# A longer unused strip ahead of the last stage's buffers

## The reference

```python
# 1: attention, 4 x 8 heads, 768 positions, head size 64
keep = is_sink | in_window            # 4 sink keys, a window of 128
a = softmax(where(keep, q @ k.T / 8, -1e9));  x = (a @ v)   # as rows [3072, 512]
# 2: routed experts, 8 of them, F = 1024, top 1, for rows with x @ w_skip > 0
y = gate_w * (relu(x @ w1[e]) @ w2[e]);       x = x + y
# 3: dense, d_ff = 2048
h = x @ w_in;  r = maximum(h, 0);  g = r * r
out = g @ w_out                       # [3072, 512] float32
```

## The kernel before

| tile | bytes | address before | address after |
|---|---|---|---|
| `to_line` | 96, then 1504 | 218,880 | 217,472 |
| `x_hi` | 8192 | 210,688 | 209,280 |
| `x_lo` | 8192 | 202,496 | 201,088 |
| `relu_c` | 4096 | 198,400 | 196,992 |
| `g` | 4096 | 194,304 | 192,896 |
| `g_hi` | 4096 | 190,208 | 188,800 |
| `g_lo` | 4096 | 186,112 | 184,704 |

## Time and profile before

### The profile page before, as it was taken

How to read it: one execution, slowest core, us unless ns; L and a number is a source line. 1 busy time by engine, 2 the same in 40 slices (tenths; PEclk the granted TensorE clock), 3 DMA queues, 4 the chain that set the end, 5 groups by cost and what they waited for, 6 DMA issues and landing times.

```text
span 937.1 us, 16992 instructions
## 1 busy us (share of the span) xinstructions
PE 914.0 (98%) x5152; PEld 731.1 (78%) x5153; DVE 472.6 (50%) x1419; ACT 420.8 (45%) x970; POOL 81.7 (9%) x147
## 2 busy tenths in 40 slices
PE   7999999989999998999999999999999999999998
PEld 5778777767888876788888887888888888878886
DVE  5787899876666767653242234222422332242224
ACT  7888999844666667542131223111311222232122
POOL 3111111123111111100000000000000000000000
PEclk9999999989999999999999999999999999999999
DMA  5556774375666688620021003000400040004001
GB/s 197 168 164 218 222 239 152 98 282 187 233 243 225 234 309 301 234 46 1 0 63 28 1 1 85 4 0 0 90 0 0 0 90 0 0 0 90 0 0 45
DMA packets 87364, 99.52 MB, mean 106 GB/s; under 512 B 56093, under 2 KB 56221, under 8 KB 87312
## 3 DMA queue, kind: packets, MB, share of 16 engines
q1 hardware_dynamic: 81168, 83.34, 28.3%
q0 software_dynamic: 6000, 15.49, 4.9%
q10 hardware_dynamic: 144, 0.07, 0.0%
HBM read 77.72 MB, written 25.56 MB: 110 GB/s over the span
## 4 chain that ended last, share of the span: by engine, by line
PE 91%; issue 2%; ACT 2%; DVE 2%; DMA 1%; ACTq 1%; DVEq 0%; SPq 0%
PE bank L1128 29%; PE bank L1114 29%; PE bank L1029 7%; PE bank L1010 7%; PE bank L869 5%; PE bank L924 4%; PE bank L897 4%; PE bank L935 1%; PE bank L1018 1%; PE bank L949 1%; PE bank L917 1%; DMA w_raw<-in_weights 1%; PE bank L1002 1%; ACT prob L667 0%; DVE x_row L1304 0%
## 5 line engine op out<-in xcount | busy, mean ns | idle before, releaser
L1498 DVE TENSOR_TENSOR g<-relu_c 128x512 f32<-128x512 f32 x96 | 66.4, 692 | 353.9 <-ACT relu_c L812 353.8
L812 ACT ACTIVATE relu_c<-bank 128x512 f32<-128x512 f32 x96 | 57.3, 597 | 385.1 <-PE bank L1114 385.1
L1114 PE MATMUL bank<-x_hi,w_lo 128*128 128x512 f32 x384 | 151.5, 395 | 0.7 <-DVE x_lo L1485 0.7
L1128 PE MATMUL bank<-w_hi,g_lo 128*128 128x512 f32 x384 | 152.0, 396 | 0.0
L1128 PE MATMUL bank<-w_lo,g_hi 128*128 128x512 f32 x384 | 151.7, 395 | 0.0
L1114 PE MATMUL bank<-x_lo,w_hi 128*128 128x512 f32 x384 | 151.6, 395 | 0.0
L1128 PE MATMUL bank<-w_hi,g_hi 128*128 128x512 f32 x384 | 151.5, 395 | 0.0
L1114 PE MATMUL bank<-x_hi,w_hi 128*128 128x512 f32 x384 | 151.5, 395 | 0.0
L667 ACT ACTIVATE prob<-score,neg_max 128x264 f32<-128x264 f32 (+1 forms) x192 | 94.0, 496 | 15.0 <-DVE neg_max L1190 15.0
L1457 DVE TENSOR_TENSOR w_lo<-w_raw,w_hi x70 | 81.9, 1220 | 21.3 <-ACT w_hi L775 10.3
L1128 PEld LDWEIGHTS bank<-w_hi,g_lo 128*128 128x128 f32 x384 | 72.1, 188 | 18.8 <-DVE g_lo L1505 1.6
(11 more groups left out here) (149 smaller groups left out, 1282.1 us busy)
## 6 DMA issues: line engine op xcount, KB each, us to landing
w_raw<-in_weights SPq DMA_DIRECT2D x80, 512.0 KB, 5.0
k_in<-in_kT SPq DMA_DIRECT2D x24, 264.0 KB
q_in<-in_qT SPq DMA_DIRECT2D x24, 256.0 KB, 3.4
v_in<-in_v SPq DMA_DIRECT2D x24, 256.0 KB
x_rows<-x_row SPq DMA_DIRECT2D x24, 256.0 KB
x_row<-x_rows SPq DMA_DIRECT2D x96, 64.0 KB, 2.4
out<-w_raw SPq DMA_DIRECT2D x12, 512.0 KB, 2.9
x_res<-routed POOLq DMA_DIRECT2D x15, 260.0 KB, 3.3
```

Of the source, the lines that this page charges most:

```text
L1114: ins = eng.matmul(hc_ps[f % 2][:, :], w[f // UNIT][:, f % UNIT, wcols], x[:, c, :], start=(c == 0 and n == 0), stop=(c == DC - 1 and n == 2))
L1128: ins = eng.matmul(yc_ps[s][:, :], gg[:, f % 2, s * P:(s + 1) * P], w[f // UNIT][:, f % UNIT, DM:CH], start=(f == 0 and n == 0), stop=(f = ...
L1498: eng.tensor_tensor(g[:, f % 2, :], relu_c[:, f % 2, :], relu_c[:, f % 2, :], ALU.mult).then_inc(s_cg, 1)
```

## The change

The strip's length is written down as 1504 bytes; before, it was worked out as 128 - 32 = 96 bytes. The six tiles of the last stage move down by 1408 bytes. No instruction is added, removed or reordered.

```diff
-LINE = 128
+TO_LINE = 1504
...
         part_hi, part_lo, sits = hb_hi[:, 0, :], hb_lo[:, 0, :], hb_lo[:, 1, :]
-        sb("to_line", [P, (LINE - 8 * 4) // 4], F32, side="right")
+        sb("to_line", [P, TO_LINE // 4], F32, side="right")
         x_hi = sb("x_hi", [P, DC, SUPER], F32R, side="right")
```

## The result

The changed kernel takes 924.66 us (median of 4 runs, 922.68 to 927.08) against 937.44 for the kernel before on the same chip: a ratio of 0.9865, 95% interval 0.9847 to 0.9884, or 12.8 us less. The forecast was 922.2, in a range of 920.5 to 938.0. The profiled executions are 938.59 and 924.29 us, 14.3 apart.

The account below looks back on a forecast made before the run. It took TensorE's matmul spacing to bound the last stage: 15.4 us from 233.3 to 226.7 ns, less 0.6 for `g_lo` waits and 0.35 unsettled, gives 14.5 off 936.7, so 922.2 us, range 920.5 to 938.0.

Parts of the forecast that it names:

- the full gain: Last stage: both matmul lines settle at 226.7 ns; 14.5 us gained, 922.2 us (920.5 to 924.5), chance 0.50.
- the signs it named: Last stage: 2.72 us per 12 matmuls, some 441 per 100 us, durations 0.39, ScalarE's L1114 wait down about 14 us.
- TensorE's spacing bounds the last stage: Last stage: only the spacing of TensorE's matmuls sets the time, 233.3 ns each against 226.7 in the expert stage.
- The spacing comes from where the two operands lie: Last stage: operands start 128 bytes apart modulo 512; 256 apart, as in the expert stage, should save 6.6 ns each.
- The exchanged roles in `inner`: In `inner` (L1114) `x` moves and weights stand, unlike the expert stage; after the change its streams are also 256 bytes apart.
- Nothing: Rival: something other than the address keeps the last stage's spacing at 233.3 ns; time stays 936.7 us, chance 0.27.
- half: Rival: in the last stage only `outer` settles, gaining 3.2 to 7.6 us; 931.3 us, chance 0.13.
- slower: Rival: `inner`'s new address pair meets worse, 236 ns a matmul, 3.1 us lost; about 940 us, chance 0.10.
- The sum: Last stage: 15.4 us from faster spacing, less 0.6 for waits and 0.35 for unsettled matmuls, gives 14.5 us gained.
- the wait for `g_lo` at the end of a round: Last stage, `outer` at each round's end: one spacing 0.33 us in place of 0.23, 6 times, 0.6 us stays.
- The 0.2 us either way for ScalarE and VectorE: Their reads and writes of the six moved tiles: taken as 0, bounded by 0.2 us to either side.

Follow-up runs that it names:

- the run with `g_lo` first: Changed kernel with VectorE's last `lower_part` of a round moved ahead of `turn_c` for the fourth chunk: 921.38 us against the changed kernel's 923.52.
- the second timing: The changed kernel, unaltered, timed once more against the kernel before on one chip: 923.52 us against 936.73, ratio 0.9861.

## Why the prediction was right

The range of 920.5 to 938.0 us held both the full gain and no change at all, so that the time fell into it says little. What bears the prediction out is the signs it named, above all 2.72 us for 12 matmuls in both lines and 441 of them in 100 us. Its ground was one difference between two stages and its chance for the full gain 0.50; that the address was the right one among the differences was shown only by the experiments.

*TensorE's spacing bounds the last stage.* Right: groups of 12 matmuls went from 2.80 us to 2.72 and the stage shrank by 13.34 us, with nothing else changed.

*The spacing comes from where the two operands lie.* Right, and shown by moving the weights alone. The prediction was wider than it had to be: it said that only a dependence on the remainder modulo 512 or a smaller power fits, and it is the smaller power 256. What it argued from, that the rhythm doesn't follow c or s, couldn't tell the two apart, since a slice is 512 bytes. The exchanged roles in `inner`, on which it doubted, make no difference at a multiple of 256 bytes, but at 64 bytes the direction counts. The strip of 1504 bytes works because it brings the tiles to a multiple of 256 from the weights; 224 bytes do the same, and the tiles need not lie as the expert stage's do.

*Nothing, half, slower.* "Nothing" fell: the same matmuls take 2.80 or 2.72 us for 12 by placement alone. The Trainium skill (TensorE: Matmul & The Clock Gate, "Step-by-step: what each phase is for") says that loading the next tile's weights takes no read bandwidth from the running matmul. The measurement decides against the conclusion that placement therefore costs nothing; whether read bandwidth is what is lost, or something else on the way of the two operands, no run shows. "Half" exists, but only where the tiles of the two layers lie at different distances. The price named for "slower", 236 ns a matmul, was never met over a group: 2.80 us for 12 in the last stage, and 4.21 for 18 in the expert stage, are the dearest steady groups on the chain at any distance tried.

*The sum.* It gave 14.5 us for the stage; 13.34 came. The mis-sized term is the wait for `g_lo` at the end of a round, set at 0.10 us, 6 times. With faster matmuls TensorE reaches that point sooner after the round's last `inner`, while VectorE, which that `inner` sets going and which makes `g_lo` after two pieces of `x_lo` and two transposes, takes as long as before. Between the two lie the 24 matmuls of two `outer` groups; by an estimate from the spacings they take 24 x 6.6 ns = 0.16 us less, and the wait for `g_lo` grew from 1.6 to 2.5 us over 6 rounds, by 0.15 each. So the two spacings of 0.38 and 0.34 are 0.15 and 0.11 above 0.227, 6 x 0.27 = 1.6 us, where 0.6 was left. That is 1.0 of the 1.1 us missing, and the run with `g_lo` first got back 1.79 us of the stage (524.37 - 522.58). The prediction asked what the faster engine would reach too early in the middle of the round, where there are 3.5 us to spare; at its end it took the wait as it stood. The 0.2 us either way for ScalarE and VectorE held: `x_lo` still takes 674 ns.

*The time.* 922.2 stands 2.5 us below the measured 924.66, which is just outside the bounds given for the full gain (920.5 to 924.5); the second timing, 923.52, is inside. Of the 2.5, 0.7 is that the kernel before was taken at 936.7 where four runs gave 937.44, and 1.1 is the sum's. The rest is that the medians differ by 12.8 us (13.2 in the second timing, 936.73 - 923.52) where the stages differ by 13.3, which is within what the runs vary.

## What to carry to other kernels

When two stretches of the same matmul form run at the same granted clock with different spacing, and no wait on the chain explains it, compare where their stationary and moving operands start: here 6.6 ns of 233.3 hung on it, 13.3 us in 2304 matmuls, and unused bytes bought it back. For this form of matmul, place the two operands' tiles a whole number of 256 bytes apart, by a strip on one side, with slices that are multiples of that; tiles placed for one stage can spoil another that shares the weights. After a bound engine gets faster, look again at the end of each loop, where the slack is least: here what was queued ahead of the last value that it waits for was worth some 2 us.

## What the runs showed of the hardware

The spacing of 128x128 by 128x512 FP32R matmuls, each with its own weight load, settles at 226.7 ns at full clock if both operands start 0 or 256 bytes apart modulo 512. It is about 233 if they start 128 apart modulo 256. It is also about 233 at 32 apart to either side and with a moving operand 64 bytes below the stationary one, and 230 to 233 with a moving operand 64 bytes above, all these with tiles off a multiple of 128 bytes.

At half the clock the placement costs nothing in the one place that shows it. Early in the expert stage nine matmuls of `layer1` run at a granted clock of 0.50 (1.2 GHz). The chain has the kernel before, distance 256, and then the run with the weights moved, distance 384:

```profile
194.88 3.84 PE bank L1010 x9
194.78 3.84 PE bank L1011 x9
```

That is 426.7 ns each at both distances, where the same line at full clock takes 4.08 and 4.20 us for 18.

The spacing settles, and not at once: after a wait some seven to fourteen matmuls go by at 231 to 236 ns even in the fast case. At the head of the changed kernel's last stage the 13 spacings from 394.72 to 397.72 us are 231 ns each, and 24 matmuls take 5.77 us, 0.33 above 24 x 0.2267 (0.11 of it in the first spacing, 394.38 to 394.72).

That the placement of the two operands sets the spacing is shown. That their reads meet somewhere is only the likeliest reading of it: no run here changed the width of an operand or read one without the other, so neither that nor the unit of memory is shown. Nor is it shown why a slow line beside a fast one spoils some of its gain.
